# First batch's attention in two parts of its queries, query blocks of 58 with 64 keys, token chunks of 432

## What is computed

```python
# q, k, v: (4 batches, 8 heads, 576 tokens, 64)
q_d, k_d, v_d = (t.reshape(B, H, 144, 4, D).mean(axis=3) for t in (q, k, v))
out_up = repeat(softmax(q_d @ k_d.T / 8) @ v_d, 4)         # coarse: 144 x 144 per head
mask = abs(pos[:, None] - pos[None, :]) < 4                  # local: 7 keys per query
out_local = softmax(where(mask, q @ k.T / 8, -1e9)) @ v
x = (out_up + out_local) as (2304 tokens, 512)
h = maximum(maximum(x @ w1, x @ w2), x @ w3)                 # 512 -> 768
y = h @ w_out                                                # 768 -> 512
out = maximum(0.01 * (y @ w_in), y @ w_in) @ w2_out          # 512 -> 2048 -> 512
```

## Time and profile before

| | us |
|---|---|
| median of 3 runs | 866.97 |
| lowest, highest | 866.44, 867.93 |
| the profiled execution, its own time | 866.58 |
| its span in the profile | 864.8 |
| first matmul of the first layer starts at | 84.87 |
| mean granted PE clock, share of full speed | 0.982 |

### The profile page before, as it was taken

How to read it: one execution, slowest core, us unless ns; L and a number is a source line. 1 busy time by engine, 2 the same in 40 slices (tenths; PEclk the granted TensorE clock), 3 DMA queues, 4 the chain that set the end, 5 groups by cost and what they waited for, 6 DMA issues and landing times.

```text
span 864.8 us, 14430 instructions
## 1 busy us (share of the span) xinstructions
PE 810.5 (94%) x6000; PEld 754.1 (87%) x6000; DVE 359.2 (42%) x654; ACT 261.7 (30%) x546; POOL 111.8 (13%) x80
## 2 busy tenths in 40 slices
PE   3545899999999999999999999999999999999997
PEld 2434799999999999999999999999999999999996
DVE  7576563566546653433223223223223223223222
ACT  2433322332222423233234423223223223223221
POOL 3453231111111011002124510000000000000000
PEclk9995799999999999999999999999999999999999
DMA  8632111122221111014008102002002002000000
GB/s 276 239 95 75 42 57 45 57 85 58 60 83 47 52 30 43 2 61 151 28 4 257 48 1 73 0 0 73 0 0 73 0 0 73 0 0 36 0 0 37
DMA packets 27886, 48.82 MB, mean 56 GB/s; under 512 B 2272, under 2 KB 17632, under 8 KB 27840
## 3 DMA queue, kind: packets, MB, share of 16 engines
q1 hardware_dynamic: 27840, 48.16, 17.5%
HBM read 38.72 MB, written 9.44 MB: 56 GB/s over the span
## 4 chain that ended last, share of the span: by engine, by line
PE 89%; DVE 7%; issue 2%; ACT 1%; POOL 1%; ACTq 0%; POOLq 0%; DVEq 0%
PE mlp_ps L534 19%; PE mlp_ps L536 19%; PE mlp_ps L535 19%; PE att_ps L601 8%; PE att_ps L600 8%; PE att_ps L599 8%; PE att_ps L505 2%; PE att_ps L526 2%; PE att_ps L470 2%; PE att_ps L498 1%; PE att_ps L516 1%; DVE prob_g L801 1%; PE att_ps L486 1%; DVE row_sum L790 1%; DVE row_sum L793 1%
## 5 line engine op out<-in xcount | busy, mean ns | idle before, releaser
L534 PE MATMUL mlp_ps<-x_hi,wa_lo 128*128 128x288 f32 (+1 forms) x792 | 246.6, 311 | 1.0 <-DVE x_lo L823 1.0
L535 PE MATMUL mlp_ps<-x_lo,wa_hi 128*128 128x288 f32 (+1 forms) x792 | 243.5, 307 | 0.0
L536 PE MATMUL mlp_ps<-x_hi,wa_hi 128*128 128x288 f32 (+1 forms) x792 | 243.4, 307 | 0.0
L534 PEld LDWEIGHTS mlp_ps<-x_hi,wa_lo 128*128 128x128 f32 x792 | 150.0, 189 | 6.3 <-issue 3.2
L535 PEld LDWEIGHTS mlp_ps<-x_lo,wa_hi 128*128 128x128 f32 x792 | 150.1, 190 | 2.4
L536 PEld LDWEIGHTS mlp_ps<-x_hi,wa_hi 128*128 128x128 f32 x792 | 149.9, 189 | 0.0
L873 DVE TENSOR_TENSOR h_raw<-mlp_ps,half_max 128x384 f32<-128x384 f32 x96 | 53.6, 558 | 211.3 <-ACT half_max L718 211.3
L718 ACT ACTIVATE half_max<-mlp_ps 128x384 f32<-128x384 f32 x96 | 47.2, 492 | 200.3 <-PE mlp_ps L536 200.3
L877 DVE TENSOR_TENSOR h_lo<-h_raw,h_hi 128x384 fp32r<-128x384 f32 x96 | 55.7, 580 | 56.9 <-ACT h_hi L695 56.9
L695 ACT ACTIVATE h_hi<-h_raw 128x384 fp32r<-128x384 f32 x96 | 50.5, 526 | 59.9 <-DVE h_raw L873 59.9
L601 PE MATMUL att_ps<-wa_hi,h_hi 128*128 128x512 f32 x162 | 64.0, 395 | 0.0
(11 more groups left out here) (92 smaller groups left out, 1207.8 us busy)
## 6 DMA issues: line engine op xcount, KB each, us to landing
qk_in<-in_qk SPq DMA_DIRECT2D x16, 576.0 KB, 4.5
v_win<-in_v_band SPq DMA_DIRECT2D x16, 315.0 KB
v_rows<-in_v_sum SPq DMA_DIRECT2D x16, 288.0 KB
wa_raw<-in_w SPq DMA_DIRECT2D x6, 768.0 KB, 6.9
y_scratch<-y_out SPq DMA_DIRECT2D x32, 144.0 KB, 1.8
x_raw<-y_scratch SPq DMA_DIRECT2D x6, 768.0 KB, 4.7
out<-o_stage SPq DMA_DIRECT2D x18, 256.0 KB, 2.1
wa_raw<-in_w_in SPq DMA_DIRECT2D x9, 256.0 KB, 4.6
```

What stands on the lines that cost most here:

```text
L534: nc.tensor.matmul(ps, wlo, xhi, start=(n == 0), stop=False)
L535: nc.tensor.matmul(ps, whi, xlo, start=False, stop=False)
L536: last = nc.tensor.matmul(ps, whi, xhi, start=False, stop=(n == len(pairs) - 1))
```

## The change

1. **Blocks of 58.** Local blocks have 58 used queries (of 64 computed) and 64 keys in place of 64 and 70. There are 10 blocks; mask and probabilities have 10 slots of 64 in place of 9 of 70. The slots are laid out so that two of them side by side transpose as one 128 x 128 (5 transposes for 9), and the keys of a block lie on the upper or lower 64 rows. `values` goes round four quarters of the array: key rows 0-63 or 64-127, head rows 0-63 or 64-127.
2. **Two parts in batch 0.** A unit is (pair, part). Batch 0's four pairs have a FRONT part, 6 blocks and 87 coarse queries (348 tokens), and a BACK part, 4 blocks and 57 coarse queries; the others stay WHOLE. There are 20 units. All FRONT units stand ahead of the first group, each followed by its `("X", 0, kk)`, the split of 288 tokens. The BACK units stand in chunk 0's groups. FRONT units use the four banks of the first layer too.
3. **Chunks.** The first layer works on chunks of 288, 288 and four times 432 tokens, each with 18 h and 4 y groups (`NM` = 22), in that order.
4. **Order.** WHOLE units now have 5.5 groups each, in chunks 1, 2 and 3; one group stands between N and T. Chunks 4 and 5 have no attention beside them.
5. **Smaller edits.** ACT and DVE take the coarse scores first, then the local ones; POOL splits a weight tile of 1536 columns in 4 parts of 384; k and q swap places; the first loads are in another order; the output stage shares `x_raw`'s first half.

```diff
-TQ = 64
-NT = S // TQ
-WIN = TQ + 2 * (FACTOR - 1)
+TQ = 64
+NT = 10
+STEP = TQ - 2 * (FACTOR - 1)
+USED = [(0, STEP)] * (NT - 1) + [(STEP * (NT - 1) - (S - TQ), TQ)]
...
+PART_MASK = {WHOLE: (0, 5), FRONT: (0, 3), BACK: (3, 5)}
+PART_GROUPS = {WHOLE: ((0, 72), (72, 72)), FRONT: ((0, 87),), BACK: ((87, 57),)}
+UNITS = ([(p, FRONT) for p in range(PAIRS)] + [(p, BACK) for p in range(PAIRS)]
+         + [(p, WHOLE) for p in range(PAIRS, NPAIR)])
...
+CHUNK = [(0, 288), (288, 288)] + [(S + 432 * i, 432) for i in range(4)]
+GROUPS = [("h", f, w) for f in range(NF1) for w in range(3)] + [("y", f, 0) for f in range(KM)]
...
+    v = {3: 0, 4: 4.5, 5: 9, 6: 13.5, 7: 17.5}
+    v.update({WHOLE0 + PAIRS * i + j: NM * (i + 1) + 0.5 + 5.5 * j for i in range(B - 1) for j in range(PAIRS)})
+    for u in range(BACK0, NU):
+        before = v[u - 1]
+        if u > BACK0:
+            s_at = max(v[u - 2] - 2, 1)
+            put(s_at - 1, ("D", u))
+            put(s_at, ("S", u))
+            put(s_at + 1, ("E", u))
...
+        put(before + 1, ("N", u))
+        put(before + 2, ("T", u))
+        put(v[u], ("V", u))
...
-LT = ((0, 3), (3, 6), (6, 9))
-AV = ((0, 5), (5, 9))
+LT = {WHOLE: ((0, 3), (3, 5)), FRONT: ((0, 3),), BACK: ((0, 2),)}
...
+FRONT_BANK = {"dt0": 4, "lt0": 5, "up": 4, "av0": 6, "av1": 7}
...
+                while any(queues.values()):
+                    for r, h in ((0, 0), (1, 1), (0, 1), (1, 0)):
...
+                        rows, keys = slice(h * D, (h + 1) * D), slice(r * TQ, (r + 1) * TQ)
...
+                        last = nc.tensor.matmul(bank(f"av{r}", u)[rows, at0:at0 + q1 - q0],
+                                                v_win[keys, u % 2, v_index(part, r, t), rows],
+                                                probT_l[keys, n // 2, half * TQ + q0:half * TQ + q1],
+                                                start=True, stop=True)
```

More of the change, by code:

```diff
@@ L20 @@
 NPAIR = B * PAIRS
-TQ = 64
-NT = S // TQ
-WIN = TQ + 2 * (FACTOR - 1)
-WIN_START = [min(max(TQ * t - (FACTOR - 1), 0), S - WIN) for t in range(NT)]
+SCALE = float(D) ** -0.5
+MASKED = -1.0e30
 SD = S // FACTOR
@@ L110, with x_home @@
-FIRST = first_phase()
-JOB_BANK = {"sl0": 0, "sl1": 1, "sg0": 2, "sg1": 3, "dt0": 0, "dt1": 1, "lt0": 2, "lt1": 3, "lt2": 0,
-            "up": 1, "av0": 2, "av1": 3}
-STAGE_JOBS = {"S": ("sl0", "sl1", "sg0", "sg1"), "T": ("dt0", "dt1", "lt0", "lt1", "lt2"), "V": ("up", "av0", "av1")}
+NG = NC1 * NM
+HG = 3 * NF1
+def x_home(b):
+    return (b + 1) % 2
+SEGMENTS = []
+for _t0, _n in CHUNK:
+    _segs, _t = [], _t0
+    while _t < _t0 + _n:
+        _m = min(_t0 + _n, (_t // S + 1) * S) - _t
+        _segs.append((_t // S, _t % S, _t - _t0, _m))
+        _t += _m
+    SEGMENTS.append(_segs)
@@ L119, with combines, build @@
     for _kind in STAGE_JOBS.get(_item[0], ()):
-        _job = (_kind, _item[1])
+        if _kind in ("dt1", "lt1") and UNITS[_item[1]][1] != WHOLE:
+            continue
+        _job, _bank = (_kind, _item[1]), bank_of(_kind, _item[1])
         JOB[_job] = len(JOB)
-        BEFORE[_job] = _last.get(JOB_BANK[_kind])
-        _last[JOB_BANK[_kind]] = _job
-JOBS = len(JOB)
-LT = ((0, 3), (3, 6), (6, 9))
-AV = ((0, 5), (5, 9))
[L130 to L142, removed]
+        BEFORE[_job] = _last.get(_bank)
+        _last[_bank] = _job
+    if _item[0] == "M":
+        BEFORE[_item] = _last.get(BANKS + _item[1] % BANKS)
+        _last[BANKS + _item[1] % BANKS] = _item
+JOBS = len(JOB)
+LT = {WHOLE: ((0, 3), (3, 5)), FRONT: ((0, 3),), BACK: ((0, 2),)}
+def combines(part):
+    out = []
+    for r, (both, one) in enumerate(PART_OUT[part]):
+        out.append((r, both, None))
+        if one is not None:
+            out.append((r, (one,), r))
+    return out
+COMBINED = [sum(len(combines(part)) for _, part in UNITS[:u]) for u in range(NU + 1)]
+EVACS = [sum(sum((_k, _u) in JOB for _k in STAGE_JOBS["T"]) for _u in range(_n)) for _n in range(NU + 1)]
+HIGH_AT = {GROUPS.index(("h", f, 2)) + 1: f for f in range(NF1)}
+LOW_AT = {GROUPS.index(("h", f, 2)) + (2 if f != NF1 - 1 else 1): f for f in range(NF1)}
+W_PARTS = [KM] * NF1 + [1] * NF1
+W_LOW = [sum(W_PARTS[:c]) for c in range(NW + 1)]
+def build(nc, kq, v_sum, v_band, w123, w_out, v_in, v_out, out, y_dram):
     with ExitStack() as ctx:
@@ L454, in _, with begin @@
         def _(pe):
-            def begin(kind, p):
-                before = BEFORE[kind, p]
+            def begin(job):
+                before = BEFORE[job]
                 if before is not None:
@@ L509, in values @@
-            def values(p):
+                        n = place(part, h, bp)[1]
+                        last = nc.tensor.matmul(ps[h][half * TQ:(half + 1) * TQ, n * TQ:(n + 1) * TQ],
+                                                q[rows, Q_START[t]:Q_START[t] + TQ], k[rows, W_START[t]:W_START[t] + TQ],
+                                                start=True, stop=True)
+                        if t == blocks[-1]:
+                            last.then_inc(att_done, 1)
+                pe.wait_ge(sums_ready, u + 1)
@@ new lines, in scores @@
+                begin(("sg0", u))
+                begin(("sg1", u))
+                gs = [bank("sg0", u), bank("sg1", u)]
+                kd, qd = kq_sum[:, p % PAIRS, 0:SD], kq_sum[:, p % PAIRS, SD:2 * SD]
+                tiles = PART_GROUPS[part]
+                for n, (q0, nq) in enumerate(tiles):
+                    for h in range(2):
+                        rows = slice(h * D, (h + 1) * D)
+                        last = nc.tensor.matmul(gs[h][:nq, n * SD:(n + 1) * SD], qd[rows, q0:q0 + nq], kd[rows, :],
+                                                start=True, stop=True)
+                        if n == len(tiles) - 1:
+                            last.then_inc(att_done, 1)
@@ L510, in values @@
+            def values(u):
+                p, part = UNITS[u]
+                tiles = PART_GROUPS[part]
+                nq = sum(n for _, n in tiles)
                 pe.wait_ge(vmean_ready, p + 1)
-                pe.wait_ge(probT_evac, 5 * p + 5)
-                ps = begin("up", p)
+                pe.wait_ge(probT_evac, EVACS[u + 1])
+                begin(("up", u))
+                ps = bank("up", u)
                 for kt in range(KT):
@@ L650, in h_high, with exps @@
-            def h_high(half, f, b):
-                act.wait_ge(h_raw_ready, 2 * NF1 * b + NF1 * half + f + 1)
-                nc.scalar.activation(h_hi[:, f * HALF:(f + 1) * HALF], h_raw[:, f % 2, 0:HALF], ACT.Copy
+            def exps(u):
+                part = UNITS[u][1]
+                tiles, n = PART_GROUPS[part], 2 * len(PART_SLOTS[part][0])
+                glob = prob_g[:tiles[0][1], u % 2, 0:2 * len(tiles), :]
+                act.wait_ge(shifted, 2 * u + 1)
+                nc.scalar.activation(glob, glob, ACT.Exp, scale=SCALE / FACTOR ** 2).then_inc(exp_done, 1)
+                act.wait_ge(shifted, 2 * u + 2)
+                local = prob_l[:, u % 2, 0:n, :]
+                nc.scalar.activation(local, local, ACT.Exp, scale=SCALE).then_inc(exp_done, 1)
```

791 lines of the change are left out of this document (427 added, 364 removed), and 5 rows, old and new, of the table items.

## The result

| | before | after |
|---|---|---|
| median of the runs, us | 866.71 | 840.94 |
| lowest, highest | 866.38, 867.93 | 839.58, 843.14 |
| the profiled execution: time, span | 866.58, 864.8 | 839.58, 837.8 |
| first matmul of the first layer at | 84.87 | 42.60 |

The account below looks back on a forecast made before the run. PE was taken to bound the kernel, busy 770.97 of 779.93 us from 84.87 us on. Span 864.8 - 42.4 + 8.0 + 1.5 - 7.0 - 2.0 + 6.9 = 829.8, with 1.8 and 0.4 832 us; range 821 to 850.

Parts of the forecast that it names:

- Section 1: Front: FRONT units at 8.0 us of DVE each; first layer's start counts as 42.5 against 84.87, -42.4 us.
- Section 2: Behind the start: BACK units' S, T and V on PE +8.0 us; first WHOLE unit's S, formerly ahead, +1.5.
- Section 3: 12 WHOLE units beside the first layer: cheaper local T and V, 0.5 to 0.65 us less per unit, -7.0.
- Section 4: First layer's matmuls: four chunks of 432 columns for six half batches of 288, -2.0 us, bounds -4 and 0.
- Section 5: PE's waits behind the start: 14.5 us of new waits at T, y and BACK units, 7.6 go: +6.9.
- What goes: ... 5.6. With 2.0 of the rest, 7.6 goes: Old waits behind the start: 5.6 us at the unit after the first groups and 2.0 others vanish, 7.6 together.
- no net change: First layer's PE clock: matmuls at 1.2 GHz after a thin stage once or twice as before, no net change.
- Late FRONT: Rival, front: FRONT stage keeps more of its chain, 10.5 us per unit, start 10 later, 842 us; chance 0.14.
- DVE late everywhere: Rival, WHOLE units: double attention density makes every T and V wait 1.2 us more in 12 units, 846; chance 0.14.
- Quarters: Rival, local V: quarters don't overlap or each mode change drains, -7.0 becomes about 0, 839 us; chance 0.07.
- The slower case: Rival, WHOLE units: waits at T bring the low clock each time, about 60 us more, 892 us; chance 0.05.
- several stretches of the low clock after 60 us: Sign of being wrong, PE after 60 us: several low-clock stretches; beside a start beyond 50 or V at 1.3.

Follow-up runs that it names:

- Experiment 4: The changed kernel with POOL's sums of v ahead of the weight split, twice in the FRONT stage: 834.89 us, 0.9657 of the kernel before.
- Experiment 8: Changed kernel with WHOLE units' T one group later, N behind the last h split at two units, and eight chunks of 288: 837.94 us, 0.9667 of the kernel before.
- experiment 11: The kernel before, with V of the previous unit moved behind N for units 1 to 3 of the first batch: 867.91 us, ratio 1.0009.
- experiment 1: The changed kernel with T of each WHOLE unit one group later, so two groups stand between N and T: 837.26 us, 0.9653 of the kernel before.
- whole_t_h: Changed kernel with batch 0's units WHOLE ahead of the first group, T one group later, N behind the h split at two units: 829.01 us, 0.9553 of before.
- whole_spread_t_h: As whole_t_h, with batch 1's four units at groups 4.5, 17, 26 and 39, also taking the BACK units' room: 827.94 us, 0.9545 of the kernel before.

## Why the prediction was right in direction and 9 us short

- **Section 1, the start: right**, 42.60 for 42.5, though in part by luck. DVE's stages of a FRONT unit take 7.5 us and not 8.0 (D 1.0, S 2.1, N 2.3, V 0.9, X 1.2), and the T stages, at 14.36, 21.34, 30.20 and 34.60, are 7.0, 8.9 and 4.4 apart and not 8 each. In return PE waited 2.46 and 2.86 us for POOL's `v_mean`, which stood behind a weight split; the second wait left DVE idle for 2.62 us ahead of the last V, where the sum had 0.9 for `upT`. Experiment 4 took this away and the start came to 40.08.
- **Section 2: BACK units right, the other term half of what it should be.** By the distances of the matmuls around them, S took 0.72, T 0.61 and V 0.85 each: 3 S, 4 T and 4 V are 8.0. But "The first WHOLE unit's S stood ahead of the start", +1.5, counts one S too few. The kernel before has six S ahead of 84.87 us (at 5.09, 9.63, 24.02, 41.33, 58.65 and 75.96), so those of two units of batch 1; the S in its order list under "The change" is that of the second of them, not of the first. Now the S of all twelve WHOLE units stand behind the start, two more than before, which is 2.9 us.

```profile
58.65 1.44 PE L470 MATMUL att_ps<-qk_in 64*64 64x70 f32 x36 [0.62 <-issue]
75.96 1.32 PE L470 MATMUL att_ps<-qk_in 64*64 64x70 f32 x36 [0.62 <-issue]
```

- **Section 3, WHOLE units: right, a little low.** By the same distances V costs 1.57 (before 1.78), T 0.96 where it didn't wait (before 1.41), S 1.47 (before 1.50), so 0.69 per unit and 8.3 in twelve, for 7.0. Local V reads 0.91 as forecast. V was forecast at 1.48, and 0.3 more would have made it 1.78; so a change of mode cost 0.1 here at the most, and the rival built on it falls. The Trainium skill (TensorEngine Tiling (Array Packing), Key Properties) states that a change of tiling mode drains TensorE. No drain is visible in this trace: the coarse part of a V runs from 121.47 for 0.71 us and the local part starts at 122.11.
- **Section 4, chunks: nearly twice the forecast.** 432 columns are 0.1956 apart (612 matmuls from 309.80 to 429.52, below) as forecast, but over long stretches of the kernel before 288 columns are 0.1325 (452 matmuls from 378 to 438 us), not the 0.1317 that the earlier trace rows had from one short one. 1728 x 0.1325 less 1152 x 0.1956 is 3.6, for 2.0 (1728 x 0.1317 less 1152 x 0.196 is 1.8). Experiment 8 has 4.6 in the spans.

```profile
309.80 0.35 PE L679 MATMUL mlp_ps<-h_hi,wo_lo 128*128 128x432 f32 x1
...
429.52 0.35 PE L679 MATMUL mlp_ps<-h_hi,wo_lo 128*128 128x432 f32 x1
```

- **Section 5, the waits: the step that failed.** The list of new waits was good where it was worked out: T of WHOLE units 6.2 (1.68, 0.74, 0.73, 1.09, 1.95) for 4.2 + 2.0, the y groups 4.1 for 4.4. Three things were wrong around it.
  First, "What goes: ... 5.6. With 2.0 of the rest, 7.6 goes". The whole first layer had 4.5 us idle before; the 8.96 hold 4.5 of the second layer too, which stayed. Of the 5.6, 3.7 were idle (2.28, and 0.84 and 0.62 inside T and S) and 1.8 were matmuls that ran slowly, while the new waits were counted by idle time alone; and the "2.0 of the rest" can have been no more than 0.8. Compared like with like, the term is 14.5 - 4.5 = 10.0 and not 6.9; 11.5 was measured. Restarts come on top of idle time, but they are not new: a T that waited takes 0.45 to 0.47 more than its wait and 0.96 (the five of WHOLE units: blocks of 3.10, 2.17, 2.15, 2.50 and 3.36 us), and in the kernel before six T's cost 1.89 to 1.93 against 1.41 with no wait in their rows. That is 2.3 us now and 3.0 before.

  Second, BACK units waited 5.5 and not 2.4. N of such a unit is short, but beside POOL's weight split, now in four pieces, its last steps took 0.92 and 1.21 where 0.44 and 0.40 would do (0.5 and 0.8 more; beside one whole piece a step took up to 2.8 more, experiment 11), and its S follows T with no group between, so it waited 0.56 for ACT. DVE's and POOL's timelines, then PE's:

```profile
59.37 0.92 DVE L965 TENSOR_TENSOR prob_g<-prob_g,row_inv 57x288 f32<-57x288 f32 x1
60.22 1.21 DVE L967 TENSOR_TENSOR prob_l<-prob_l,row_inv 128x256 f32<-128x256 f32 x1
```

```profile
57.04 4.10 POOL L552 TENSOR_TENSOR wa_lo<-wa_raw,wa_hi 128x384 fp32r<-128x384 f32 x4 [0.54 <-ACT wa_hi L834]
```

```profile
60.35 0.39 PE L620 MATMUL att_ps<-ident,prob_g 57*72 57x57 f32 x4 [1.25 <-DVE prob_g L965]
61.48 0.64 PE L629 MATMUL att_ps<-ident,prob_l 128*128 128x128 f32 x2 [0.74 <-DVE prob_l L967]
62.68 0.71 PE L588 MATMUL att_ps<-x_raw 64*64 64x64 f32 x16 [0.56 <-ACT probT_l L789]
```

  Third, "no net change" of the clock. Matmuls stood at the distances of 1.2 GHz in four stretches (42.6 to 44.5, 60.9 to 68.3, 232.1 to 235.7, 259.7 to 262.6), against two before (84.9 to 90.5, 97.3 to 104.2). By what the same instructions need at 2.4 GHz I estimate 7 us lost for 5.8. Of the three behind the start one follows the three waits of 2.55 us together shown above, the others one of 1.74 and one of 1.95. Yet a wait alone doesn't decide it: in this profile those of 1.68 and 2.38 us (at 113.67 and 157.75) are followed by full pace.

In numbers, behind the start: 15.3 us measured (14.0 and 1.25) for 7.4 forecast, 7.9 more. Idle 4.6, the second S of section 2 1.4, the second layer 1.25 and the clock about 1.2 add; chunks 1.6, WHOLE units 1.3 and the restarts of T 0.7 take back. That leaves about 3 us unassigned. The second layer's 1.25 is not explained either; its idle time is the same in both (4.4 and 4.5).

**The rivals.** Late FRONT: no. DVE late everywhere: no; from 85 to 165 us it is 77% busy, and the waits stand at five T's, not at each. Quarters: no. The slower case: its mechanism is there, at three places instead of twelve. One of the prediction's own signs of being wrong came true, "several stretches of the low clock after 60 us"; the start and the local V came as it said.

## What to carry to other kernels

When waits of before and after are set against each other, count both in one way: idle time plus what the restart and the low clock cost behind it. Count which stages stand ahead of a boundary from the trace, not from the plan: here one S was missed. A wait that is ended by another engine moves to the next stage that shares its buffers unless work stands between (experiment 1). Before a gain of some us is read from one profile each, compare where both ran at the low clock. And before work is cut in two to start a stage earlier, try the kernel without the cut: here, with the same order and instructions otherwise, it was as fast.

## What was not expected of the hardware

- The same 40 quarter matmuls take 0.91 us going round all four quarters, with the two PSUM banks in turn, and 1.42 with the key rows, and so the banks, one after the other.
- A DVE step of 13 elements took 0.17, 1.09 or 2.94 us, by where in POOL's 3.42 us it fell.
- A low clock in a thin stage cost little. Ahead of the first layer, nearly every matmul of `whole_t_h` and `whole_spread_t_h` takes the same long time (40 local scores 1.35 us, where they take 0.81 beside the first layer), although the clock column reads 1.00 for the first 56 us of the one and 0.76 for the other. Only between 22 and 29 us do they differ. V of `whole_t_h`, and the T behind it:

```profile
23.12 1.23 PE L646 MATMUL mlp_ps<-probT_g,v_mean 72*64 72x144 f32 x8
24.27 1.53 PE L669 MATMUL mlp_ps<-probT_l,v_win 64*64 64x58 f32 x40
28.86 0.70 PE L621 MATMUL mlp_ps<-ident,prob_g 72*72 72x72 f32 x4 [3.06 <-DVE prob_g L966]
```

  The same place of `whole_spread_t_h`:

```profile
22.64 0.71 PE L646 MATMUL mlp_ps<-probT_g,v_mean 72*64 72x144 f32 x8
23.28 0.91 PE L669 MATMUL mlp_ps<-probT_l,v_win 64*64 64x58 f32 x40
28.56 0.50 PE L621 MATMUL mlp_ps<-ident,prob_g 72*72 72x72 f32 x4 [4.37 <-DVE prob_g L966]
```

  PE is through with V some 1.6 us earlier in the second, waits 1.3 us longer for DVE, and the first layer starts 0.3 us earlier (55.64 for 55.95).
